# Attention and two expert mixtures on one core: where the router's small products stand among TensorE's work in the first mixture

## The reference

```python
x = attn_out.transpose(0, 2, 1, 3).reshape(2304, 512)
# first mixture
expert_idx = argmax(x @ w_gate); gate_w = softmax(x @ w_gate)[expert_idx]
pos[i] = rows before i with the same expert; keep[i] = pos[i] < capacity
out[i] = gate_w[i] * (relu(x[i] @ w1[e]) @ w2[e])      # 512 -> 1024 -> 512
# second mixture, on the rows y = out of the first
do_compute = y @ w_skip > 0
e_idx, gate_w from y @ w_gate2, as above, without a capacity
out = y + gate_w * (relu(y @ w1b[e]) @ w2b[e])  where do_compute, else y
```

## Time and profile before

| what | us |
|---|---|
| median of 3 runs (lowest, highest) | 682.29 (681.94, 683.03) |
| the profiled execution, its own time | 680.41 |
| its span, from first to last instruction | 678.9 |
| TensorE busy with matmuls | 661.6 |
| VectorE busy | 370.6 |
| ScalarE busy | 299.0 |
| GpSimd busy | 205.6 |

### The profile page before, as it was taken

How to read it: one execution, slowest core, us unless ns; L and a number is a source line. 1 busy time by engine, 2 the same in 40 slices (tenths; PEclk the granted TensorE clock), 3 DMA queues, 4 the chain that set the end, 5 groups by cost and what they waited for, 6 DMA issues and landing times.

```text
span 678.9 us, 17205 instructions
## 1 busy us (share of the span) xinstructions
PE 661.6 (97%) x5640; PEld 580.6 (86%) x5641; DVE 370.6 (55%) x1029; ACT 299.0 (44%) x713; POOL 205.6 (30%) x329
## 2 busy tenths in 40 slices
PE   7999999999998999999999999999999999999997
PEld 6788888788787889998899888888899899899996
DVE  3776878887787743367633367434711453411144
ACT  3777877878785122244422244123222352311233
POOL 5633436436343213222222212222122131112112
PEclk7999999999999999999999999999999999999999
DMA  8766567556515148410711148882364778701101
GB/s 175 186 186 184 149 178 228 149 123 206 118 35 173 69 117 307 183 39 24 257 53 40 47 165 315 322 304 78 129 239 158 277 277 316 262 31 48 45 18 34
DMA packets 95616, 105.91 MB, mean 156 GB/s; under 512 B 63757, under 2 KB 63757, under 8 KB 95568
## 3 DMA queue, kind: packets, MB, share of 16 engines
q1 hardware_dynamic: 84608, 81.03, 38.3%
q0 software_dynamic: 8912, 22.36, 9.8%
q10 hardware_dynamic: 2048, 1.87, 0.9%
HBM read 83.44 MB, written 28.63 MB: 165 GB/s over the span
## 4 chain that ended last, share of the span: by engine, by line
PE 92%; DVE 4%; issue 2%; ACT 1%; DVEq 0%; another core or an unknown queue 0%; POOL 0%; ACTq 0%; POOLq 0%
PE ps L1568 32%; PE ps L1576 26%; PE ps L1463 8%; PE ps L1414 6%; PE ps L1438 5%; PE ps L1390 3%; PE ps L1470 3%; PE ps L1540 2%; PE ps L1404 2%; PE ps L1546 1%; PE ps L1431 1%; PE ps L1554 1%; PE ps L1381 1%; DVE negmax L815 0%; PE ps L1419 0%
## 5 line engine op out<-in xcount | busy, mean ns | idle before, releaser
L1568 PE MATMUL ps<-xT,w 128*128 128x128 f32 x1344 | 159.5, 276 | 1.2 <-issue 1.0
L1568 PEld LDWEIGHTS ps<-xT,w 128*128 128x128 f32 x1344 | 155.2, 192 | 5.0 <-issue 3.0
L1576 PE MATMUL ps<-w_hi,hT_hi 128*128 128x512 f32 x256 | 104.7, 409 | 0.9 <-DVE hT_lo L1084 0.7
L1576 PE MATMUL ps<-w_lo,hT_hi 128*128 128x512 f32 x256 | 100.3, 392 | 0.0
L1576 PE MATMUL ps<-w_hi,hT_lo 128*128 128x512 f32 x256 | 99.7, 389 | 0.0
L1295 ACT ACTIVATE hT_hi<-ps 128x512 fp32r<-128x512 f32 x64 | 37.9, 592 | 116.6 <-PE ps L1568 116.6
L1568 PE MATMUL ps<-xT,w_last 128*128 128x128 f32 x704 | 86.3, 277 | 0.0
L1568 PEld LDWEIGHTS ps<-xT,w_last 128*128 128x128 f32 x704 | 82.3, 192 | 2.9 <-issue 2.1
L1084 DVE SCALAR_TENSOR_TENSOR hT_lo<-ps,hT_hi 128x512 fp32r<-128x512 f32 x64 | 44.2, 691 | 63.6 <-ACT hT_hi L1295 60.1
L1290 ACT ACTIVATE w_hi<-w2all 128x1024 fp32r (+1 forms) x48 | 47.0, 1046 | 62.8 <-PE ps L1576 56.9
L542 POOL DMA_INDIRECT out<-xs,idxo x32 | 37.3, 1165 | 110.4 <-DVE xs L1117 102.8
(11 more groups left out here) (200 smaller groups left out, 1050.0 us busy)
## 6 DMA issues: line engine op xcount, KB each, us to landing
w2all<-in_moe_w SPq DMA_DIRECT2D x10, 2048.0 KB, 14.6
w<-in_moe_w SPq DMA_DIRECT2D x7, 2048.0 KB, 9.4
rows<-queue POOLq DMA_DIRECT2D x36, 257.0 KB, 3.0
w2all<-in_moe_w SPq DMA_DIRECT2D x16, 512.0 KB, 4.8
w<-in_moe_w SPq DMA_DIRECT2D x12, 512.0 KB, 3.7
w_last<-in_moe_w SPq DMA_DIRECT2D x3, 2048.0 KB
qn<-in_q SPq DMA_DIRECT2D x32, 144.0 KB, 5.1
out<-pad SPq DMA_DIRECT2D x4, 1152.0 KB
```

What stands on the lines that cost most here:

```text
L1568: last = mm(hTp[j // 4][:, j % 4, :], w1s[slot][:, c, j * P:(j + 1) * P], xT[:, c, :], start=(c == 0), stop=(c == DC - 1))
L1576: last = mm(yp, h_[:, j, :].bitcast(f32r), w_[:, j, :].bitcast(f32r), start=(j + n == 0), stop=(j == FC - 1 and n == 2))
```

## The change

Three calls are moved on TensorE; nothing is added or removed, and no other engine's program changes.

- In every tile of the first mixture but tile 0, `add_logits` goes from between hidden 6 and hidden 7 to behind hidden 7.
- In the same tiles `ranks_y` goes from behind values 0 to behind values 2.
- At the border `last_ranks` goes from behind hidden 2 to behind hidden 3.

```diff
                         hidden(range(4, 6), slot)
                         chunk_logits(t)
-                        hidden(range(6, 7), slot)
+                        hidden(range(6, FC), slot)
                         add_logits(t)
-                        hidden(range(7, FC), slot)
...
                     values_here(t, 0)
-                    values_of(range(0, 1))
+                    values_of(range(0, 3))
                     if phase == 0:
                         ranks_y(t)
-                    values_of(range(1, 4))
+                    values_of(range(3, 4))
                     values_here(t, 1)
...
                     last_logits(total)
-                    hidden(range(2, 3), 0)
+                    hidden(range(2, 4), 0)
                     last_ranks(total)
-                    hidden(range(3, FC), 0)
+                    hidden(range(4, FC), 0)
```

## The result

Over 8 runs the changed kernel takes 684.77 us (683.29 to 688.9), beside 682.32 us (681.04 to 683.03) for the kernel before: a ratio of 1.0040, with an interval of 1.0021 to 1.0058. That is 2.4 us slower where 1.2 was forecast: within the range, but above the 0.2% taken as the bound of "no change".

A forecast was written before the change was run, and what follows sets the result against it. TensorE, carrying 92% of the chain of waits, was taken as the bound, including its queue's waits and table reads. Terms 0.5 + 0.16 + 0.89 - 0.31 = +1.2 us gave 683.5 us, range 682.2 to 685.4.

The forecast's parts named there:

- the remainder makes every tile wait: Rival: values 4 of 15 loop tiles wait for VectorE's second-half remainder, 0.1 to 0.15 us each; 684.4 to 685.1; chance 0.12.
- Loop tiles, 14 x 0.035 us: Values 4 load 0.36 us behind VectorE's later remainder, losing about 0.035 us in each of 14 tiles: 0.5 us.
- Tile 1, +0.16: In tile 1 values 4 start later because the remainder ends later: cost 0.16 us, bounds 0 and 0.3.
- Tile 11, +0.89: At tile 11's end TensorE's queue passes the remainder's wait later, then reads three expert counts: +0.89 us, bounds 0.8 and 1.0.
- Tile 12, -0.31: At tile 12's end TensorE arrives later, so its wait for weights from memory goes: -0.31 us, bounds -0.31 and 0.
- The clock rival, chance 0.08: TensorE's clock halves after the longer gap near 398 us, perhaps only in some executions: 685.2 to 686.9; chance 0.08.
- clock not 1.00 around 400 us: A sign named beforehand: the prediction is wrong if the clock around 400 us is not 1.00.
- The border, 0: At the border the ranks' idle 0.71 us goes, but values 0 wait about 1.2 us, starting as before: worth 0.
- the ranks, 0: Ranks moved behind values 2 never wait, but in the loop did not wait before either; no cost of their own.
- The rival of cheaper ranks: Ranks' load comes less late in 16 tiles, gaining up to 0.16 us each: 680.3 us; chance 0.05.
- Idle time not tied to the remainder: Rival: tile 11's queue table reads wait for something else, leaving 0.5 to 0.7 us of small waits: 682.9; chance 0.07.

The follow-up runs named there:

- e_before: The kernel before, unchanged, run and traced a second time: 681.69 us, ratio 0.9989.
- e_before2: The kernel before, unchanged, once more on the same chip as a repeat of the changed kernel: 681.84 us, ratio 1.0007.
- e_ranks: The kernel before with only the tiles' ranks moved behind values 2, sum and border as before: 682.44 us, ratio 1.0000.
- e_border: The kernel before with only the border's ranks moved behind hidden 3: 682.34 us, ratio 0.9992.
- first sample: The changed kernel's original 8 runs and profile, against the kernel before: 684.77 us, ratio 1.0040.
- e_loop: The changed kernel without its border part (border's ranks back between hidden 2 and 3), against the kernel before: 684.26 us, ratio 1.0035.
- e_after: The changed kernel, unchanged, run again for a second trace and time, 12 runs against the kernel before: 680.74 us, ratio 1.0028.
- e_after2: The changed kernel, unchanged, once more on the same chip as a repeat of the kernel before: 683.89 us, ratio 1.0040.
- e_split_onehot: The changed kernel with VectorE's remainder of the second half moved right behind the one-hot rows, 0.5 us sooner: 681.91 us, ratio 1.0004 against the kernel before.
- e_delay_before: The kernel before with four small VectorE instructions ahead of the remainder, making it 0.76 us later, TensorE unmoved: 679.29 us, ratio 1.0010.
- e_delay_after: The changed kernel with one more small VectorE instruction (some 0.2 us) ahead of the remainder: 684.07 us, ratio 1.0084 against the kernel before.
- second series: The runs that delayed or advanced the remainder, plus a repeat of the changed kernel, against the kernel before on their own chip (678.43 us there).

## Why the prediction was right or wrong

The mean over tiles 3 to 16 is 203.94 us for the five profiled executions without the late sum (before, e_before, e_before2, e_ranks, e_border). It is 205.02 for the two of the changed loop at full clock, 206.62 for the two where the clock fell, and 205.82 over all four. So 1.1 us is the change at full clock and, if the clock falls in half of the executions as in these four, 0.8 the clock; with 0.15 at tile 1 it is about 2.0 us, of 2.4 measured. The rest lies inside the interval of the ratio (1.4 to 4.0 us).

That the forecast had the 1.1 us for these tiles is in part luck. Two sizes were wrong and cancel: the 12 loop tiles cost 0.8 us at full clock where 0.42 was summed, tiles 11 and 12 together 0.26 where it was 0.58. And 684.77 us lies in the band of the rival *the remainder makes every tile wait* (684.4 to 685.1), though the tiles lost 0.06 to 0.08 us and not the 0.1 and more that this band was worked out from.

- **Loop tiles, 14 x 0.035 us.** The mechanism and the delay were right: 0.36 us were assumed from remainder to load, and 0.36 measured. The size was wrong. A tile lost 0.06 to 0.08 us: over the 12 tiles 3 to 10 and 13 to 16, the changed kernel's first sample is 0.96 us longer than the kernel before's (116.08 + 58.01 against 115.51 + 57.62), e_loop 0.67, e_after 0.82, e_after2 0.74. The second matmul of values 4 runs 11.98 us into the tile, where before it ran at 351.94 + 0.23 - 340.23 = 11.94: 0.04 us where the sum had 0.03. Behind it the matmuls come (358.14 - 355.62) / 11 = 0.229 us apart and not 0.227, which gives the rest (e_loop: 11.97 us and 0.228). The step stopped at the first late matmul. Beside e_split_onehot (14.41 us), which has the same order on TensorE with the remainder in time, the lateness costs 0.06 to 0.09 us a tile.
- **Tile 1, +0.16.** Right in the three executions of the changed loop that have a partner with the same tile 0: 14.64 or 14.65 us against 14.49 or 14.50. Tile 0 took 14.0 to 16.3 us whatever the kernel, and tile 1 varies with it: where it took 14.0, the kernel before had 15.14 and e_after 14.78, which no run explains.
- **Tile 11, +0.89.** Measured 0.86 to 0.91 on 15.81. Right, and e_delay_before shows the cause by itself.
- **Tile 12, -0.31.** Right in kind and undersized where the clock held: 14.38 us in both such executions, beside 14.64 to 15.31 (mean 15.01). The four other executions without the late sum waited longer for the weights than the one I read, so the recovery was 0.3 to 0.9 us. Where the clock fell it turned into a loss: 16.00 us.
- **The clock rival, chance 0.08.** This is the weakest step. The rival had the place (tile 11's gap), the price (1.7 us at least; 5.46 - 3.83 = 1.63 measured) and "only some executions". Its chance was taken as if it were a case beside the forecast, when a fall in a large share of the executions moves the median too. Two of four profiled executions of the changed loop had it, none of the five without the late sum. By my own test (clock not 1.00 around 400 us) the forecast was wrong in those two. The Trainium skill (TensorE: Matmul & The Clock Gate, "What's actually happening") has the gate go back to half after idleness; these two traces agree. Three with a gap of the same length (the first sample, e_loop and e_delay_after) show no fall.
- **How often it falls** is not shown. The first sample's profiled execution kept its clock and took 684.75 us, where the median of the eight is 684.77. The mean granted clock of each run is only a hint, since it doesn't tell where the clock was low. The two values that went with a fall there in the profiles (0.997 without, 0.992 with the low stretch at the start) came in 18 of 32 runs of the changed loop (3 of 8, 8 of 12, 5 of 6, 2 of 6) and in 20 of 120 runs without the late sum, 5 of them in the ten of e_ranks, where no gap grew. In the second series the times go with it (median 681.13 us for the eight, 679.57 for the other four, 678.43 before), in the first sample and in e_loop they don't.
- **The border, 0, and the ranks, 0.** Right: e_border and e_ranks show nothing, and e_loop shows the whole cost without the border. The rival of cheaper ranks fell: their load comes as late as before.
- **Idle time not tied to the remainder.** Fell: 5.18 to 5.21 us lie between the two in the kernel before, the changed one, e_delay_before and e_split_onehot. That each tile waits 0.1 us or more for the remainder does not hold of the changed kernel (0.06 to 0.08 on average), but one instruction more on VectorE makes it so (e_delay_after).

What stays open: why the clock falls in some executions and not in others behind a gap of the same length. e_loop and e_after2 idled 1.87 and 1.85 us; only one fell. e_delay_after, at 1.81 us, and e_delay_before, at 1.74, kept their clock in their one profile each, and none of e_delay_before's ten runs had either of the two values. No run varied the length of the gap alone with enough profiles to count falls, so that the gap is the cause is the likeliest reading, not shown.

## What to carry to other kernels

Ask of a wait not only which matmul it holds back, but what the queue has to do behind it: register work and table reads that are hidden in most tiles cost in full where a group ends, and the last of several waits starts them. A gap on TensorE that grows can have a second price in the clock, paid in a share of the executions; put an estimate of that share into the sum, and profile more than one execution before calling the clock steady. Where a load comes late, count the matmuls behind it too, and before delaying what a wait needs, check with one small added instruction how much delay is still free.

## What the runs showed of the hardware

- The clock fell to half for 3.4 us, beginning 0.9 us (e_after) or 1.2 us (e_after2) after TensorE had resumed from an idle time of 1.8 us, in two of the five executions with such a gap (not in the first sample, e_loop and e_delay_after). The 32 matmuls behind that gap took 1.63 us longer.
- After a late weight load, fp32 matmuls of 512 columns came 0.228 (e_loop) to 0.229 us (the first sample) apart over the next eleven instead of 0.227, so the tile lost more than its first late matmul did.
- Three expert counts read by TensorE's queue, with the jumps over two experts, took 5.2 us from the end of the last wait's work to the next product, in four kernels (5.18 to 5.21).
- A bfloat16 weight load between values matmuls came after 0.26 us in which no weights were loaded, though its data had been there for 1.7 us (e_ranks).
